# Clustered attention with two feed-forward blocks: keys split one step earlier, the last part of the one-hot work on VectorE

## What is computed

```python
q_assign = argmax(einsum('bhsd,hcd->bhsc', q_n, c_n))      # nearest of 16 centroids, by cosine
k_assign = argmax(einsum('bhsd,hcd->bhsc', k_n, c_n))
mask = q_assign[:, :, :, None] == k_assign[:, :, None, :]
scores = where(mask, q @ k.T / 8, -1e9)
x = softmax(scores) @ v                                     # then heads side by side: (1536, 512)
h = x @ w_in;  g = (a0 + a1 h + a2 h^2 + a3 h^3) / (1 + |b0||h| + |b1| h^2 + 1e-6);  x = g @ w_out
h = x @ w2_in; out = (h - tanh(h)) @ w2_out
```

## Time and profile before

| | us |
|---|---|
| runs shown (median of 3) | 838.07 (837.94 to 838.96) |
| the profiled execution: its own time | 838.88 |
| its span, first to last instruction | 837.1 |
| TensorE matmul busy | 794.2 (95%) |
| VectorE busy | 519.9 (62%) |
| ScalarE busy | 503.0 (60%) |
| GpSimd busy | 374.1 (45%) |

### The profile page before, as it was taken

The page is one execution under the profiler, slowest core; times in us unless marked ns, Lnnn a source line. Parts: engine busy times, 40 slices in busy tenths (PEclk is TensorE's granted clock), DMA queues, the critical chain, the costliest instruction groups (busy, mean ns, idle before and its releaser), DMA issues.

```text
span 837.1 us, 11654 instructions
## 1 busy us (share of the span) xinstructions
PE 794.2 (95%) x4066; PEld 681.7 (81%) x4066; DVE 519.9 (62%) x868; ACT 503.0 (60%) x954; POOL 374.1 (45%) x419
## 2 busy tenths in 40 slices
PE   6889999899997889999999999999999999999998
PEld 6788888888887877788788888888888888888886
DVE  4588788887888869999987787996401111111111
ACT  3578788787887867887867677777522222222222
POOL 4477877878778843222222222224722222222222
PEclk9999999999999999999999999999999999999999
DMA  4632322323221023200000002114200100001001
GB/s 127 174 81 62 93 74 62 82 62 92 66 63 43 15 77 113 92 23 1 0 1 1 1 25 76 51 50 125 77 1 0 39 13 1 0 1 51 1 0 51
DMA packets 39082, 41.17 MB, mean 49 GB/s; under 512 B 4720, under 2 KB 30320, under 8 KB 39024
## 3 DMA queue, kind: packets, MB, share of 16 engines
q1 hardware_dynamic: 39024, 40.42, 17.3%
HBM read 26.25 MB, written 3.15 MB: 35 GB/s over the span
## 4 chain that ended last, share of the span: by engine, by line
PE 66%; DVE 17%; POOL 10%; ACT 3%; issue 2%; DMA 1%; SPq 0%; DVEq 0%; POOLq 0%; ACTq 0%
PE y_ps L1068 26%; PE h_ps L1047 25%; PE s_ps L974 4%; POOL probs L407 4%; PE pv_ps L1004 3%; PE pt_ps L987 2%; PE pr_ps L934 2%; DVE pt_lo L795 2%; DVE nmax L782 2%; DVE f_bc L848 2%; DVE f_t L867 2%; DVE w_lo L822 2%; DVE f_bc L865 2%; DVE f_a L861 1%; POOL nk L424 1%
## 5 line engine op out<-in xcount | busy, mean ns | idle before, releaser
L509 POOL TENSOR_TENSOR g_lo<-f_t,g_hi 128x512 fp32r<-128x512 f32 x96 | 125.0, 1302 | 377.8 <-ACT g_hi L605 377.8
L902 DVE TENSOR_TENSOR f_t<-h_ps,f_a 128x512 f32<-128x512 f32 x48 | 33.2, 691 | 203.4 <-ACT f_a L684 203.4
L1047 PE MATMUL h_ps<-x_hi,w_hi 128*128 128x512 f32 x384 | 149.5, 389 | 1.3 <-DVE w_lo L822 1.3
L1047 PE MATMUL h_ps<-x_lo,w_hi 128*128 128x512 f32 x384 | 149.5, 389 | 0.0
L1047 PE MATMUL h_ps<-x_hi,w_lo 128*128 128x512 f32 x384 | 149.4, 389 | 0.0
L605 ACT ACTIVATE g_hi<-f_t 128x512 fp32r<-128x512 f32 x96 | 60.8, 633 | 138.9 <-PE y_ps L1068 123.5
L568 ACT ACTIVATE pt_hi<-pt_ps 128x384 fp32r<-128x384 f32 x192 | 85.1, 491 | 55.4 <-PE pt_ps L987 54.3
L407 POOL TENSOR_SCALAR probs<-probs,rinv 128x768 f32<-128x768 f32 x96 | 86.1, 908 | 59.0 <-DVE rinv L789 58.8
L795 DVE TENSOR_TENSOR pt_lo<-pt_ps,pt_hi 128x384 fp32r<-128x384 f32 x192 | 99.0, 550 | 21.7 <-ACT pt_hi L568 21.0
L782 DVE TENSOR_REDUCE nmax<-s_ps 128x1 f32<-128x768 f32 x96 | 91.2, 950 | 17.3 <-PE s_ps L974 17.2
L561 ACT ACTIVATE probs<-s_ps,nmax 128x768 f32<-128x768 f32 x96 | 86.7, 903 | 3.4 <-DVE nmax L782 3.4
(11 more groups left out here) (125 smaller groups left out, 1583.5 us busy)
## 6 DMA issues: line engine op xcount, KB each, us to landing
w_raw<-in_moe_w_in_dram SPq DMA_DIRECT2D x32, 256.0 KB, 2.9
w_raw<-in_moe_w_out_dram SPq DMA_DIRECT2D x32, 256.0 KB, 3.4
ka<-qk_b SPq DMA_DIRECT2D x32, 192.0 KB, 3.0
raw_q<-in_q_dram SPq DMA_DIRECT2D x16, 192.0 KB, 2.6
raw_k<-in_k_dram SPq DMA_DIRECT2D x16, 192.0 KB, 2.8
raw_v<-in_v_dram SPq DMA_DIRECT2D x16, 192.0 KB, 3.0
qk_b<-qa SPq DMA_DIRECT2D x16, 192.0 KB, 2.7
out_dram<-f_bc SPq DMA_DIRECT2D x12, 256.0 KB, 2.1
```

The lines of the kernel that those rows point to most:

```text
L509: pool.tensor_tensor(g_lo[n % 2][:, :], f_t[n % 2][:, :], g_hi[n % 2][:, :].bitcast(F32), ALU.subtract).then_inc(g_lo_done, 1)
L902: dve.tensor_tensor(f_t[n % 2][:, :], h_ps[n % 4][:, :], f_a[n % 2][:, :], ALU.subtract).then_inc(g_done, 1)
L1047: last = pe.matmul(h_ps[n % 4][:, :], w[f][:, ws], x[:, cols], start=(kt == 0 and i == 0), stop=(kt == KT - 1 and i == 2))
```

## The change

On GpSimd `split_k` moves from r = 2 to r = 1 and `rank_hot` from r = 1 to r = 2 (behind it now, and ahead of the scaling of r = 2). `finish_hot` leaves GpSimd; VectorE does it at r = 3, behind `read_top2` and `row_max`, in the form in which the first two heads were made: two comparisons and one multiplication on 128x96 each. `read_top2` now links. The semaphores `hot_first` and `top2_done` go. Weight chunks: ScalarE rounds chunk 0 at k = 78 instead of 79 and chunk 1 at 80 instead of 82; GpSimd splits chunks 0 to 3 at 79, 83, 85 and 91 instead of 80, 84, 86 and 90.

```diff
-        ACT_CHUNK_AT = {79: 0, 82: 1, 84: 2, 88: 3, 94: 4}
-        POOL_CHUNK_AT = {80: 0, 84: 1, 86: 2, 90: 3}
+        ACT_CHUNK_AT = {78: 0, 80: 1, 84: 2, 88: 3, 94: 4}
+        POOL_CHUNK_AT = {79: 0, 83: 1, 85: 2, 91: 3}
...
-            def finish_hot(g):
-
-                pool.wait_ge(top2_done, g - FIRST + 1)
-                pool.wait_ge(prep_done, prepared(g - 1, HOT))
-                link(pool.tensor_tensor(hot_nat[:, :, :].rearrange("p a (t c) -> p (a t) c", c=C), hot[:, :, :],
-                                        top2[:, :].unsqueeze(2).broadcast_to([P, 2 * T, C]), ALU.subtract))
-                pool.tensor_scalar(hot_nat[:, 0, :], hot_nat[:, 0, :], -1.0, 1.0, ALU.max, ALU.add).then_inc(hot_done, 1)
-                pool.tensor_scalar(hot_nat[:, 1, :], hot_nat[:, 1, :], -1.0, BIG, ALU.max, ALU.mult).then_inc(hot_done, 1)
...
-                if r == 1 and 2 <= (k + 11) // T < HEADS:
-                    rank_hot((k + 11) // T)
-                if r == 2 and 3 <= (k + 16) // T < HEADS:
-                    split_k((k + 16) // T)
+                if r == 1 and 3 <= (k + 17) // T < HEADS:
+                    split_k((k + 17) // T)
+                if r == 2 and 2 <= (k + 10) // T < HEADS:
+                    rank_hot((k + 10) // T)
                 if r == 3 and 1 <= (k + 3) // T < HEADS:
                     split_v((k + 3) // T)
-                if r == 4 and 2 <= (k + 8) // T < HEADS:
-                    finish_hot((k + 8) // T)
...
                 dve.wait_ge(hot_ranked, g - FIRST + 1)
-                dve.reduce_max(top2[:, :], hot[:, :, :], AX.X).then_inc(top2_done, 1)
+                link(dve.reduce_max(top2[:, :], hot[:, :, :], AX.X))
+
+            def finish_hot(g):
+
+                if g > 0:
+                    dve.wait_ge(prep_done, prepared(g - 1, HOT))
+                q_nat, k_nat = (hot_nat[:, i, :].rearrange("p (t c) -> p t c", t=T) for i in range(2))
+                link(dve.tensor_tensor(k_nat, hot[:, T:2 * T, :],
+                                       top2[:, T:2 * T].unsqueeze(2).broadcast_to([P, T, C]), ALU.not_equal))
+                dve.tensor_scalar(hot_nat[:, 1, :], hot_nat[:, 1, :], -BIG, None, ALU.mult).then_inc(hot_done, 1)
+                dve.tensor_tensor(q_nat, hot[:, 0:T, :], top2[:, 0:T].unsqueeze(2).broadcast_to([P, T, C]),
+                                  ALU.is_equal).then_inc(hot_done, 1)
...
                 if k + LOOK < TILES:
                     row_max(k + LOOK)
+                if r == 3 and 2 <= (k + 9) // T < HEADS:
+                    finish_hot((k + 9) // T)
...
                 elif u == HOT:
-                    if g < FIRST:
-                        pe.wait_ge(hot_first, 2 * (g + 1))
-                    else:
-                        pe.wait_ge(hot_done, 2 * (g - FIRST + 1))
+                    pe.wait_ge(hot_done, 2 * (g + 1))
```

More of the change, by code:

```diff
@@ L179, in clustered_attention_then_two_ffns @@
         max_done, rinv_done, pt_lo_done = sem("max_done"), sem("rinv_done"), sem("pt_lo_done")
-        sim_read, top_done, top2_done, xf_done = sem("sim_read"), sem("top_done"), sem("top2_done"), sem("xf_done")
-        hot_first, k_lo_first, prep_copied_dve = sem("hot_first"), sem("k_lo_first"), sem("prep_copied_dve")
+        sim_read, top_done, xf_done = sem("sim_read"), sem("top_done"), sem("xf_done")
+        k_lo_first, prep_copied_dve = sem("k_lo_first"), sem("prep_copied_dve")
         dve_chain = sem("dve_chain")
@@ L770, in first_hot @@
                 link(dve.reduce_max(top2[:, :], hot[:, :, :], AX.X))
[L771 to L778, removed]
+                finish_hot(g)
             def row_max(m):
```

## The result

| | before | after |
|---|---|---|
| median of the runs | 838.39 us (837.94 to 838.96, 4 runs) | 823.32 us (822.86 to 823.63, 4 runs) |
| the profiled execution: time, span | 838.88, 837.1 us | 823.63, 821.8 us |
| GpSimd busy | 374.1 us | 353.0 us |
| VectorE busy | 519.9 us | 526.7 us |

The ratio is 0.9819 (95% interval 0.9802 to 0.9836): 15.1 us faster, where 12.6 had been forecast. A second copy of the changed kernel, run later beside its own runs of the kernel before, took 821.75 us (820.74 to 822.40, 4 runs), ratio 0.9799 (0.9785 to 0.9812). So the change is worth 15 to 17 us.

A forecast was written before the change was run, and what follows sets the result against it. The bound was taken to be the order on GpSimd inside a closed loop of GpSimd, TensorE and VectorE. Gains of 10.8 + 0.6 + 1.2 = 12.6 us gave 826.3 profiled, 825.5 median, range 823 to 835.

The forecast's parts named there:

- Keys before ranks: GpSimd, split_k first: TensorE's 1.40 us key wait goes, 0.41 returns as probs, 0.99 us saved a head.
- The piece on VectorE: One-hot work on VectorE at r = 3, starting at 149.40: three instructions costing 0.9 us, with waits for GpSimd.
- It just fits: VectorE's pt_low of r = 4, behind the one-hot work, is done at 151.3; TensorE asks at 151.42.
- GpSimd loses three instructions [...] so that alone gives nothing: GpSimd behind the split of v: it mostly waits for reciprocals afterwards, 1.28 us to spare, so no gain alone.
- the term of 10.8 us: 12 attention heads at 0.9 us each, bounds 0.99 and below: 10.8 us faster.
- Head 2: TensorE's 1.0 us wait for hot_nat there ends with the removed GpSimd instructions: 0.6 us, between 0.2 and 1.0.
- Weight chunks: Attention's tail: chunk 0 ahead of rank_hot starts 2.1 us sooner, freeing the 2.36 us sum: 1.2 us, bounds 0 to 2.5.
- the new wait near the end: Chunk 3, one step later, stands in the way of VectorE's last two-element sum by about 0.7 us.
- Rival A: Third (or second) one-hot instruction waits for v's subtraction: 0.15 us a head left, 835 (0.14); half the heads, 830 (0.20).
- Rival B: GpSimd keeps the port until v's subtraction ends, VectorE's one-hot work follows: 0.5 us lost a head, 843.5, chance 0.07.
- Rival C: Rival A with the tail's gain lost too, moved chunks blocking VectorE: within 1.7 us of before, chance 0.07.

The follow-up runs named there:

- the longer piece: Changed kernel with two more 128x96 instructions (comparison, multiplication into a spare tile) on VectorE ahead of finish_hot: 842.27 us, ratio 1.0039.
- The order alone: Kernel before with only split_k and rank_hot exchanged on GpSimd, finish_hot staying on GpSimd, old tables: 838.84 us, ratio 1.0003.
- the kernel whose heads collided: Changed kernel with rank_hot's last instruction behind the scaling of r = 4 and row_max ahead of read_top2: 824.8 us, ratio 0.9848.

## Why the prediction was right, and where it was off

The median, 823.3 us, lies in the range (823 to 835), near its fast end, and faster by over 0.2% had the most weight. The forecast of 825.5 was 2.2 us too slow.

**Keys before ranks.** By its steps this held to 0.02 us: the scaling stayed at 5.48 after the start of the period, TensorE's r = 4 came at 6.44 (forecast 148.70 - 142.28 = 6.42), and 0.4 us of waiting came back as `probs`.

**The piece on VectorE.** It starts at 7.12 after the start of the period, as forecast. It takes 0.8 us and not 0.9: the multiplication waited 0.2 us for the v scaling, the third instruction nothing, and the first nothing either, where a wait for the scaling of r = 5 had been forecast. r = 5 gained 0.90 us, the forecast value. That there is hardly any slack behind it ("It just fits") was confirmed by the longer piece.

**The step that failed** is "GpSimd loses three instructions [...] so that alone gives nothing". It looked only at GpSimd's spare time at the end of the period, and asked "what is late next?" only for the scaling. Taken alone that is nearly so (0.12 us a head); beside earlier keys it is not. Those three instructions ended at 152.84, just before HOT at 152.98, which also stood right behind r = 5. HOT had two gates that opened at almost the same time. The order alone removes one, and HOT stays at 10.69; with both gone HOT came at 9.56 instead of 10.70, 1.14 us earlier, and the similarities 1.15. So a head gained 1.17 and not 0.9 us, and the term of 10.8 us measured 14.1. The missing 0.24 us a head was the gap from r = 5's transposes to HOT: 152.98 - 152.08 = 0.90 before, 145.28 - 144.62 = 0.66 after. The list of waits had not shown it. In the chain of work of the kernel before, 0.09 us of it stand as "issue":

```profile
152.24 0.66 PE pt_ps L987 x6
152.90 0.09 issue
152.98 0.39 PE pr_ps L943 x2
```

**Head 2.** 0.6 us forecast, 0.66 measured in the pair of profiles, but the clocks of the two profiles differed, so that the agreement is in part luck. Two profiles of the changed kernel differ by 0.9 us in this stretch (50.64 and 49.72). At full clock it is 51.30 and 50.83 in two kernels that are the kernel before up to this point, and 50.42 in one that is the changed kernel up to this point: 0.4 to 0.9 us. What happened there is in the rows. The wait of 1.01 us for `hot_nat` is gone, but the first comparison was issued 0.14 us behind the subtraction of v, and a part of the wait came back as `pt_lo`:

```profile
44.66 1.01 POOL L433 TENSOR_TENSOR v<-raw_v,v 128x384 fp32r<-128x384 f32 x1
```

```profile
44.80 0.99 DVE L755 TENSOR_TENSOR hot_nat<-hot,top 128x96 f32<-128x96 f32 x1
```

```profile
46.81 0.92 PE L979 MATMUL pt_ps<-ident,probs 128*128 128x128 f32 x6 [0.33 <-DVE pt_lo L788]
```

In the second copy and in the changed kernel with the old tables it was the multiplication, with 1.02 and 1.03 us, and TensorE waited 0.63 and 0.66 us.

**Weight chunks.** 1.2 us forecast; 0.5 in the shown profile, 1.8 in the second copy, whose clock stayed full there. By its first steps the forecast held in the second copy. Counted from the start of the period (248.64 there, 264.40 before), the transposes behind the chunk came at 7.21 (forecast 7.2, before 7.91) and HOT at 10.11 (forecast 10.2, before 11.84). The term was too small because more was passed on than the 1.1 us it took: the scaling six steps later (k = 84) is 1.50 us earlier. The two-element sum of 2.36 us takes 0.31, that of 0.96 us takes 0.15, and the new wait near the end is there, 0.82 us against a forecast of about 0.7:

```profile
284.89 0.82 DVE L781 TENSOR_SCALAR rsum_e<-rsum 128x2 f32<-128x2 f32 x1 [0.24 <-ACT probs L550]
```

**The rivals.** Rival A did not come about in the 12 heads: the multiplication lasts 0.40 or 0.41 us in all 13 periods from 61 us on. It did at head 2, as shown, and the runs show its price. Where the piece started otherwise, four of 12 heads lost 1.0 us to the v subtraction. The Trainium skill (SBUF — State Buffer, "Who interferes with whom") says that a VectorE instruction with two SBUF inputs, or in a mode that uses both port pairs, contends with GpSimd's reads, and that whoever issues first gets the shared pair for the whole instruction. The runs agree with it, but for one start too near to call: leads of GpSimd of 0.01 and 0.06 us cost VectorE 0.9 and 0.8 us over the instruction's time alone. Rival B did not come about either, but its threshold is near what the longer piece shows: it was to decide from a piece of 2.0 us, and the piece of 2.2 us made a head 0.17 us longer than before (211.54 against 209.53 us for 12). That it gave 842.3 us where rival B had 843.5 is in part luck, since rival B had 0.5 us a head. Rival C is out, by the interval.

## What to carry to other kernels

Where an operation has two inputs that come at almost the same time, the list of waits names only the later one; taking it away alone gains nothing. Before counting what a wait is worth, follow the next few operations of the waiting engine and put beside each the end of its *other* producers, spare or not: within a few tenths of a us they are gates too. And where VectorE and GpSimd meet with short and long instructions, one semaphore that lets the short ones go first can be worth more than a reordering: here 7 us of 825 in the kernel whose heads collided, and nothing in the one whose heads did not.

## What was not expected of the hardware

- Hundredths of a us decide a wait of a whole instruction. Listed 0.01 us behind GpSimd's subtraction, a comparison of 0.25 us took 1.11 in one kernel and 0.25 in another, so that which comes first can't be read from starts so near each other; 0.06 behind it, a multiplication of 0.21 took 1.02. A kernel can gain or lose 1 us in a head with no change in its work.
- The granted clock fell to 0.50 from about 257.5 to 261 us in the tail of one execution of the changed kernel and stayed at 1.00 in another, though TensorE had done the same work with the same waits just before (4.87 and 4.83 us busy in the six us before, waits of 0.89 and 0.77 us against 0.89 and 0.76). By the rows that fall cost 1.3 us. What decides it these runs don't show.
